# Attention and two MLPs on one core: token pieces of 128, 256, 384, 512, 512, 512 in place of 192, 384, 448, 512, 512, 256, with the weights split two slots sooner

## What is computed

```python
def _attn_ref(q, k, v):                 # 4 x 8 heads, 576 tokens, 64 wide, f32
    scores = scale * np.matmul(q, k.transpose(0, 1, 3, 2))
    kth = np.partition(scores, -top_k, axis=-1)[..., -top_k:-top_k + 1]   # top_k = 32
    scores = np.where(scores >= kth, scores, -1000000000.0)
    ...
    return np.matmul(attn, v)           # attn is the softmax of the kept scores
def _moe_ref(x, w_gate, w_val, w_out):  # x: 2304 tokens x 512; 1536 wide inside
    return ((1 / (1 + np.exp(-(x @ w_gate)))) * (x @ w_val)) @ w_out
def _moe2_ref(x, w_in, w_out):          # 2048 wide inside
    r = np.maximum(x @ w_in, 0.0)
    return (r * r) @ w_out
```

## Time and profile before

| | us |
|---|---|
| median of three runs (1307.43 to 1312.79) | 1310.2 |
| the profiled execution | 1313.2 |
| its span | 1311.4 |
| PE busy | 1208.8 (92%) |
| DVE busy | 842.9 (64%) |
| ACT busy | 807.9 (62%) |
| POOL busy | 654.1 (50%) |

### The profile page before, as it was taken

How to read it: one execution, slowest core, us unless ns; L and a number is a source line. 1 busy time by engine, 2 the same in 40 slices (tenths; PEclk the granted TensorE clock), 3 DMA queues, 4 the chain that set the end, 5 groups by cost and what they waited for, 6 DMA issues and landing times.

```text
span 1311.4 us, 22472 instructions
## 1 busy us (share of the span) xinstructions
PE 1208.8 (92%) x7744; PEld 1083.6 (83%) x7744; DVE 842.9 (64%) x1692; ACT 807.9 (62%) x1806; POOL 654.1 (50%) x619
## 2 busy tenths in 40 slices
PE   3669888878998979999999999999999999999999
PEld 2558777878998879999989888887788888887999
DVE  6886796846767765787899567677863444640121
ACT  5986766757677766765786677657764443541221
POOL 6974557655655845552674455435634431430221
PEclk9779898989999989999999999999999999999999
DMA  5894665666666476655566554554455645556998
GB/s 187 315 311 132 213 223 197 217 237 230 233 228 212 169 261 240 216 191 190 176 215 214 205 181 155 187 181 157 155 182 200 208 167 174 172 174 197 344 364 302
DMA packets 89249, 279.08 MB, mean 213 GB/s; under 512 B 9904, under 2 KB 11952, under 8 KB 89136
## 3 DMA queue, kind: packets, MB, share of 16 engines
q1 hardware_dynamic: 89136, 277.65, 61.5%
HBM read 237.24 MB, written 40.37 MB: 212 GB/s over the span
## 4 chain that ended last, share of the span: by engine, by line
PE 69%; DMA 9%; POOL 8%; ACT 7%; issue 4%; DVE 2%; SPq 1%; ACTq 0%; POOLq 0%; DVEq 0%
PE ps L486 18%; PE ps L488 17%; PE ps L487 17%; PE ps L421 4%; PE ps L405 4%; PE ps L393 4%; DMA raw<-qk_in 4%; DMA ring<-w_in 3%; PE ps L472 3%; DMA w_split<-ring 2%; POOL ring L735 2%; POOL below L740 2%; POOL klo L721 1%; POOL qkh L726 1%; PE ps L415 1%
## 5 line engine op out<-in xcount | busy, mean ns | idle before, releaser
L740 POOL TENSOR_TENSOR below<-scores,below 128x576 f32<-128x576 f32 x144 | 207.3, 1440 | 247.1 <-ACT below L538 246.8
L659 DVE MAX8 top<-work 128x8 f32<-128x576 f32 x432 | 313.1, 753 | 4.9
L486 PE MATMUL ps<-xy_hi,ring 128*128 128x512 f32 (+3 forms) x800 | 290.0, 362 | 2.5 <-POOL xy_lo L764 1.7
L488 PE MATMUL ps<-xy_hi,ring 128*128 128x512 f32 (+3 forms) x800 | 282.9, 354 | 0.0
L487 PE MATMUL ps<-xy_lo,ring 128*128 128x512 f32 (+3 forms) x800 | 282.7, 353 | 0.0
L661 DVE MATCH_REPLACE8 work<-top,work 128x576 f32<-128x576 f32 x288 | 214.0, 743 | 0.0
L486 PE MATMUL ps<-g_hi,ring 128*128 128x512 f32 (+3 forms) x560 | 202.7, 362 | 2.9 <-POOL ring L735 2.8
L488 PE MATMUL ps<-g_hi,ring 128*128 128x512 f32 (+3 forms) x560 | 197.9, 353 | 0.0
L487 PE MATMUL ps<-g_lo,ring 128*128 128x512 f32 (+3 forms) x560 | 197.9, 353 | 0.0
L486 PEld LDWEIGHTS ps<-xy_hi,ring 128*128 128x128 f32 x800 | 151.0, 189 | 22.0 <-issue 6.2
L686 DVE SCALAR_TENSOR_TENSOR full_buf<-act_buf,ps 128x512 f32<-128x512 f32 (+3 forms) x60 | 35.6, 594 | 206.8 <-PE ps L488 201.8
(11 more groups left out here) (67 smaller groups left out, 2212.0 us busy)
## 6 DMA issues: line engine op xcount, KB each, us to landing
ring<-w_split SPq DMA_DIRECT2D x318, 512.0 KB, 3.8
w_split<-ring SPq DMA_DIRECT2D x68, 512.0 KB, 3.8
ring<-w_in SPq DMA_DIRECT2D x113, 256.0 KB, 3.5
vt<-v_in SPq DMA_DIRECT2D x32, 320.0 KB, 3.4
raw<-qk_in SPq DMA_DIRECT2D x16, 480.0 KB, 4.7
raw<-qk_in SPq DMA_DIRECT2D x16, 448.0 KB, 4.3
raw<-qk_in SPq DMA_DIRECT2D x8, 576.0 KB, 6.2
raw<-qk_in SPq DMA_DIRECT2D x8, 512.0 KB, 4.5
```

Source lines behind the costliest of these rows:

```text
L486: nc.tensor.matmul(dst, w_hi, hi[:, k, 0:WIDTH[c]], start=first, stop=False)
L488: mm = nc.tensor.matmul(dst, w_lo, hi[:, k, 0:WIDTH[c]], start=False, stop=final)
L659: nc.vector.max(out=best, in_=sc if step == 0 else wk).then_inc(sel_step[t % 2], 1)
L740: nc.gpsimd.tensor_tensor(out=below[:, t % 2, :], in0=scores[:, t % 4, :], in1=below[:, t % 2, :], op=ALU.subtract).then_inc(mask_done, 1)
```

## The change

It changes the widths of the pieces, begins the splits of the first 23 weight blocks in slot 0 instead of slot 2, and has POOL do the last third of the previous slot's evacuations before it splits x, not after. Everything that is computed from the widths moves with them: groups, `HEADS_AT`, `V_AT`, `X_AT`, the shares.

```diff
-CHUNK_BLOCKS = (3, 6, 7, 8, 8, 4)
+CHUNK_BLOCKS = (2, 4, 6, 8, 8, 8)
...
 for _k in range(NPRE):
-    SPLIT_AT.setdefault(2 + _k // 2, []).append(_k)
+    SPLIT_AT.setdefault(_k // 2, []).append(_k)
...
                     normalise(UNIT_AT[s - NORM])
+                for c, n in blocks_of(SHARES[s - 1][2]) if s else []:
+                    evac(c, n)
                 for c, p in X_AT.get(s, []):
                     split_x(c, p)
-                for c, n in blocks_of(SHARES[s - 1][2]) if s else []:
-                    evac(c, n)
                 for g, h in HEADS_AT.get(s, []):
                     split_head(g, h)
```

## The result

The change makes the kernel slower: 1396.0 us median of 4 runs (1390.8 to 1397.7) against 1311.5 for the kernel before on the same chip. The ratio is 1.0635, with a 95% interval of 1.0585 to 1.0685. The forecast had the direction and less than half of the size: 1339 us, range 1285 to 1382.

A forecast was written before the change was run, and what follows sets the result against it. SP's serial loops were taken to bound pieces 0 and 1, PE all later pieces. 86 + 149 + 200 + 203 + 265 + 247 + 190 = 1340 us of span, giving a forecast of 1339 us, range 1285 to 1382.

The forecast's parts named there:

- The loop on SP: In pieces 0 and 1, SP's serial loads, waits and stores set the pace: turns of 5.7 and 8.4 us.
- PE's work and the last four pieces: From piece 2 on PE sets the pace: 203, 265, 247 and 190 us, together 905 us.
- The start: Time before the first MLP matmul: 86 us against 102.2 before, bounds 76 to 92.
- the 9 us: Added to the start for heads' transfers waited for on ACT, their POOL work and two more weight splits.
- 22.7 turns of 5.7 us: Piece 0: SP's loop, one turn per three of 68 blocks, 1.4 us plus 4.3 for the store's landing; 129 us.
- the 20 us for five pairs of heads on ACT: Piece 0: ACT waits about 4 us per pair while the next weight split stands behind it; brings the stage to 149.
- turns as long as now: Piece 0's upper bound: 168 us if SP's turns do not get shorter than in the kernel before.
- 22.7 turns at 8.4 us: Piece 1: SP's loop of load, split, store, mean of three turns, 190 us; with 10 for heads, 200.
- PE's clock: Piece 0: at a granted clock of 0.79 PE's 93 us would be 118, still hidden under SP's loop.
- Queues get longer: Rival: turns as long as now in pieces 0 and 1, start at 92; 1390 us in all, chance 0.10.
- the Trainium skill's formula: A transfer costs 2.0 us plus bytes at 436 GB/s; piece 0's turn would be 4.6 us, the sum 25 us lower.

The follow-up runs named there:

- a_ballast: The changed kernel with three more unread fp32 matmuls of 128 columns ahead of 48 of the 68 blocks of pieces 0 and 1: 1393.0 us, ratio 1.0624.
- b_rest: The changed kernel with the old widths put back, keeping the sooner weight splits and POOL's new order: 1312.2 us, 1.0006 of the kernel before.
- a_double: The changed kernel with every store of a split block issued twice, to two places, and the waits counting both: 1466.7 us, ratio 1.1191.
- mix3: The changed kernel with blocks split three ahead instead of four (AHEAD = 3) and piece 1's stores issued by POOL: 1358.1 us; same edit in kernel before: 1303.0.
- a_poolstore: The changed kernel with the 68 stores of split weights issued by POOL behind its part of the split, not by SP: 1372.5 us, ratio 1.0457.

## Why the prediction was right or wrong

**Direction: right; where the time is set: half right.** Pieces 0 and 1 don't follow PE's work (a_ballast), and the cost comes with the widths (b_rest). The loop on SP, read from the timeline of before, holds piece 0 of the changed kernel. In piece 1 the stage moves with ACT's waits for landings, a step inside that loop that the prediction priced by three quiet turns. The columns taken from there reappear in pieces 4 and 5 at PE's price, 243.6 and 189.9 us for 247 and 190.

**PE's work and the last four pieces: right.** 913.6 us for 905.

**The start: right in size, half wrong in reason.** 83.7 for 86. I put the 9 us down to POOL and to the transfers of heads, and both are in the stage's chain (the transfers of heads with 40% of it); a_double shows that SP's stores are in this stage's chain too, at 20 us for 23 more of them.

**Piece 0: the step that failed is the term "22.7 turns of 5.7 us" (129 us); it was too small.** The turn in quiet stretches is 6.3 us, and the stage divided by its turns is 7.6. Three things were left out or mis-sized, in SP's own account. The store lands in 4.9 us, not 4.3: 0.6 x 22.7 = 14 us. (The stage moved 221 GB/s against 207, but that is not shown to be the reason: in piece 1, at 231 GB/s, the same store landed in 3.0.) The stage has 112 issues of 0.43 us, and my turn held the three loads only: the 20 for heads, V, results and split blocks are up to 9 us, and I had called them hidden inside the turns. And SP still waits 10.3 us for POOL. With these the term is 162 us; the other 10 of the stage are not assigned. Against that, the 20 us for five pairs of heads on ACT are not confirmed: ACT's waits for them were 11.9 us in this stage, and they lengthen it only if they delay a split that SP waits for. The transfers of heads are 12% of the stage's chain, against 2.7% in a_ballast, whose stage is 7 us shorter; no run took them away. The bound of 168 for "turns as long as now" was the nearer value.

**Piece 1: the term "22.7 turns at 8.4 us" (190 us) failed as well, and was too small.** I averaged three turns from a quiet stretch of the kernel before; its whole stage had 233.2/22.7 = 10.3 and the changed one 9.9. I explained that excess by PE being late and let it vanish with the narrower piece. It didn't: the largest part that the runs can move is ACT's waiting for a landing, 49.9 us in 13 waits, with everything behind it. AHEAD = 3 gives 24 us of it back, mix3 34. That these waits are longer than before because PE's blocks are shorter, while the load is only one block ahead of the split, is likely and not shown.

**PE's clock: the size was right, that it hides was not settled.** It fell to 0.84 in piece 0, above the 0.79 that I had reckoned with, and to 0.86 in piece 1, of which I had said nothing. At 0.84 PE was busy 121.6 of the 172.5 us, so its work fitted in; what the lower clock adds to the waits of the others, a_ballast can't tell.

**The rivals.** "Queues get longer", which kept each turn as long as now and had a chance of 0.10, gave 1390 and came out. Its price was right where the forecast's was too kind. It took piece 0 at 168 (172.5), piece 1 at 225 (225.8) and the start at 92 (83.7). The row by which I rejected the Trainium skill's formula (DMA: Bandwidth & Descriptors, Anatomy of one DMA), by which an estimate for 512 KB is 3.2 us, decides the same way here. That page of the Trainium skill gives the formula for transfers issued by GpSimd, which I had not said. The store took 4.9 us in the changed kernel's piece 0 when SP issued it and 4.1 in a_poolstore's when GpSimd did; in piece 1 of the changed kernel it took 3.0, near the estimate.

## What to carry to other kernels

When a queue's serial loop holds a stage, take the stage's length divided by its turns, not the shortest turns of a quiet stretch; what stretches them need not be the engine that the change relieves. Making a piece narrower shrinks only what is paid by the column, and transfers, their issues and waits are paid by the block. Before betting on an engine as the bound, add idle work to it, and read how much its busy time really grew: here 63 us of matmuls cost nothing, but the higher granted clock gave half of them back. And when several edits move one wait, set the wait's change beside the stage's: in piece 1 that said more than any single run.

## What the runs showed of the hardware

- PE's granted clock rose from 0.84 to 0.98 in piece 0 when PE was given some 31 us more work there. Its busy time rose by only 12.7 us.
- The same store of 512 KB took 2.9 us in the median in piece 1 of the kernel before (226 GB/s over the stage), 3.0 in piece 1 of the changed one (231 GB/s), and 4.9 in piece 0 of the changed one (221 GB/s), where three loads are issued just ahead of it. So the rate over the stage doesn't order these landings.
- A store issued by POOL took 0.57 us of its list, against 0.43 on SP in piece 0. With 23 of them in the start, it was 11 to 12 us longer.
- An engine that comes to the split of a block before its load has landed stands still with its whole list: one such wait of ACT's, at the seam, was 12.9 us, for a load that SP issued 7.6 us after the store ahead of it.
